# Token rows in a region of DRAM per expert, scattered in three rounds, and the gates computed inside the first expert

## The reference: what is computed

```python
new_re = ar * S_re - ai * S_im
new_im = ar * S_im + ai * S_re
kv = np.einsum('bhd,bhe->bhde', k[:, :, t], v[:, :, t])
S_re, S_im = (new_re + kv, new_im)
y[:, :, t] = np.einsum('bhd,bhde->bhe', q[:, :, t], S_re)
```

```python
expert_idx = np.argmax(logits, axis=1)
...
for i in range(N):
    e = expert_idx[i]
    if counts[e] < capacity:
        disp[e, counts[e]] = x[i]
        pos[i] = counts[e]
        counts[e] += 1
        keep[i] = True
h = np.maximum(np.einsum('ecd,edf->ecf', disp, w1), 0.0)
y = np.einsum('ecf,efd->ecd', h, w2)
```

## Time and profile before

| | |
|---|---|
| median of 3 runs | 549.45 us (549.38 to 549.66) |
| the profiled execution | 548.02 us, span 546.1 us |
| TensorE, products | 467.5 us busy, 86% of the span |
| TensorE, weight loads | 417.7 us, 76% |
| VectorE | 363.7 us, 67% |
| ScalarE | 272.3 us, 50% |
| GpSimd | 42.9 us, 8% |
| moved by DMA | 63.69 MB, mean 117 GB/s |
| mean granted clock of TensorE | 0.952 |

### The profile page before, as it was taken

The page is one execution under the profiler, slowest core; times in us unless marked ns, Lnnn a source line. Parts: engine busy times, 40 slices in busy tenths (PEclk is TensorE's granted clock), DMA queues, the critical chain, the costliest instruction groups (busy, mean ns, idle before and its releaser), DMA issues.

```text
span 546.1 us, 10002 instructions
## 1 busy us (share of the span) xinstructions
PE 467.5 (86%) x3752; PEld 417.7 (76%) x3752; DVE 363.7 (67%) x624; ACT 272.3 (50%) x431; POOL 42.9 (8%) x48
## 2 busy tenths in 40 slices
PE   0538976999996029999999999999999999999995
PEld 0237755777885029999999998989998899889985
DVE  2688798678534317776777776778747787487751
ACT  5996758673446017666666664433334333334212
POOL 2000000000001890000000000000002000110002
PEclk9959999999998559999999999999999999999999
DMA  8970000000000469667666666233324333230001
GB/s 323 424 294 2 3 1 1 2 1 2 2 3 2 159 188 324 182 192 215 205 195 199 200 189 190 89 99 104 96 78 145 102 101 114 70 108 0 1 0 60
DMA packets 22178, 63.69 MB, mean 117 GB/s; under 512 B 2928, under 2 KB 4464, under 8 KB 22128
## 3 DMA queue, kind: packets, MB, share of 16 engines
q1 hardware_dynamic: 20592, 58.27, 32.6%
q0 software_dynamic: 1536, 4.74, 2.3%
HBM read 58.27 MB, written 4.74 MB: 115 GB/s over the span
## 4 chain that ended last, share of the span: by engine, by line
PE 74%; DVE 8%; DMA 5%; issue 5%; POOL 3%; ACT 2%; SPq 2%; DVEq 0%; POOLq 0%; ACTq 0%
PE banks L1152 15%; PE banks L1150 15%; PE banks L1151 15%; PE banks L1160 7%; DMA vv<-v_rows 4%; PE banks L1161 3%; PE banks L998 3%; POOL rows_by_slot L369 3%; PE banks L986 2%; PE banks L1017 2%; PE banks L989 2%; PE banks L950 2%; PE banks L1020 1%; PE banks L1144 1%; PE banks L1046 1%
## 5 line engine op out<-in xcount | busy, mean ns | idle before, releaser
L870 DVE TENSOR_TENSOR w_lo<-raw_early,w_hi 128x768 fp32r<-128x768 f32 x84 | 80.0, 956 | 31.1 <-ACT w_hi L543 30.0
L588 ACT ACTIVATE g_hi<-g_all 128x512 fp32r<-128x512 f32 x48 | 30.3, 632 | 118.4 <-DVE g_all L923 118.4
L543 ACT ACTIVATE w_hi<-raw_early 128x768 fp32r<-128x768 f32 x84 | 70.4, 843 | 33.2 <-PE banks L1161 32.7
L1150 PE MATMUL banks<-w_hi,g_hi 128*128 128x384 f32 x192 | 65.1, 339 | 0.5 <-DVE g_lo L925 0.5
L1152 PE MATMUL banks<-w_hi,g_lo 128*128 128x384 f32 x192 | 65.0, 339 | 0.0
L1151 PE MATMUL banks<-w_lo,g_hi 128*128 128x384 f32 x192 | 64.9, 338 | 0.0
L1160 PE MATMUL banks<-h_hi_lo,w_hi 128*128 128x448 f32 x192 | 64.0, 378 | 0.9 <-DVE h_hi_lo L886 0.9
L925 DVE TENSOR_TENSOR g_lo<-g_all,g_hi 128x512 fp32r<-128x512 f32 x48 | 33.3, 693 | 44.2 <-ACT g_hi L588 44.2
L1150 PE MATMUL banks<-ys_hi,w_hi 128*128 128x512 f32 x144 | 56.1, 390 | 1.2 <-DVE ys_lo L900 1.2
L1152 PE MATMUL banks<-ys_hi,w_lo 128*128 128x512 f32 x144 | 57.1, 397 | 0.0
L1151 PE MATMUL banks<-ys_lo,w_hi 128*128 128x512 f32 x144 | 56.8, 394 | 0.0
(11 more groups left out here) (166 smaller groups left out, 981.2 us busy)
## 6 DMA issues: line engine op xcount, KB each, us to landing
raw_early<-weights SPq DMA_DIRECT2D x84, 384.0 KB, 3.5
raw_late<-weights SPq DMA_DIRECT2D x28, 384.0 KB, 3.5
xq<-q_rows SPq DMA_DIRECT2D x3, 776.0 KB, 16.6
xq<-rows_by_slot SPq DMA_DIRECT2D x12, 194.0 KB, 4.5
kk<-k_rows SPq DMA_DIRECT2D x3, 768.0 KB, 18.0
vv<-v_rows SPq DMA_DIRECT2D x3, 768.0 KB, 19.4
aa<-a_re_rows SPq DMA_DIRECT2D x2, 768.0 KB, 10.5
th<-a_im_rows SPq DMA_DIRECT2D x2, 768.0 KB, 11.9
```

Of the source, the lines that this page charges most:

```text
L543: A(wh[:, slot, :], raw[slot], ACT.Copy).then_inc(w_hi, 1)
L588: A(gh[:, c % GBUF, :], gg[:, c % GBUF, :], ACT.Copy).then_inc(g_hi, 1)
L870: TT(wl[:, slot, :], raw[slot], wh[:, slot, :].bitcast(F32), ALU.subtract).then_inc(w_lo, 1)
L1150: MM(o, lhsT=whi, rhs=mhi, start=first, stop=False)
```

## The change

**Regions.** In DRAM each expert has a region of 1536 rows (`rows_by_expert`), its middle at row 768 of the region. Tokens of batch 0 are placed downwards from the middle and those of batch 1 upwards, so a token's place follows from its rank within its own batch, block by block, and later blocks don't move it. A window of 384 rows (`CAP`) that begins at the region's first used row, but at most 384 ahead of the middle, holds an expert's tokens.

**Zeros.** Rows in reach of a window must be defined: SyncE, after the loads of attention, copies the still all-zero `w0` to 768 rows in each region (8 transfers of 1.18 MB); `shift_state` waits for them, and so does the first scatter.

**Rounds.** `ROUNDS` cuts the six blocks into (0 to 3), (4), (5), that is tiles 0 to 7, 8 and 9, 10 and 11. `choose(r)` and `place(r)` on VectorE and `rank(r)` on TensorE do a round; the first two are put at steps 5 to 8 of the last frame, the third behind it. `X_IN` and `LOGITS_IN` place transposes and logits anew. GpSimd scatters each round's tiles when `routed` says so.

**Windows.** SyncE loads the first window in three parts, then chunks 6 and 7 of the weights, then windows 1 and 2; a further window ahead of each expert's weights. Two tiles of a window (256 rows) are turned and split: those of expert 0 ahead of the experts, those of e+1 inside expert e (TensorE after outputs 1 and 4, ScalarE and VectorE at chunks 3 and 6). The third tile is used by wide experts only.

**Gates.** Only `choose`, `place`, the region's ends, starts and flags stand between the last logits and the experts. The slot in sorted order, keep and gate weight are made by `gate_part(i)` in chunks 0 to 5 of expert 0 on VectorE. Gate and token number leave the rows (now 384 wide) and go through a DRAM array of two values a slot (`meta_by_slot`), scattered by twelve small transfers and loaded back at expert 4.

**Also.** Three of the six first weight splits come ahead of the first window, three behind; the memsets of `ys_hi` and `ys_lo` follow the last scatter; the results of the experts use four banks in turn instead of five.

```diff
+    FIRST = 3
+    WB = 4
+    MID = S
+    REGION = S + S
+    WT = CAP // P
+    NTILES = 2
+    ZT = 8
+    PADE = E // 2
+    ROUNDS = ((0, NB - 2), (NB - 2, NB - 1), (NB - 1, NB))
...
+        X_IN = {2: ((0,), (1,), (2,)), 3: ((3,), (4,), (5,)), 4: ((6,), (7,), ()), 5: ((), (), (8,)),
+                7: ((9,), (), ()), 8: ((), (), (10,)), 10: ((11,), (), ())}
+        LOGITS_IN = {2: ((), (0,), (1,)), 3: ((2,), (3,), (4,)), 4: ((5,), (6,), (7,)),
+                     6: ((), (), (8,)), 7: ((), (9,), ()), 9: ((10,), (), ())}
         assert NT == 12
+        NEXT_FROM = (1, 4)
+        NEXT_AT = (3, 6)
...
-            sp.wait_ge(bases, 1)
+            sp.wait_ge(consts, 1)
+            for e in range(E):
+                sp.dma_start(xs_dram[e * REGION + MID - CAP:e * REGION + MID + CAP, :].rearrange(
+                    "(p t) w -> p t w", t=ZT), w0[0:2 * CAP // ZT, None, 0:UW].to_broadcast([2 * CAP // ZT, ZT, UW])
+                    ).then_inc(zeroed, 16)
+
+            def window_row(e):
+                return sp.value_load(start_i[0:1, e:e + 1], min_val=0, max_val=E * REGION - CAP)
+
+            def window_rows(row, lo, n):
+                return xs_dram[bass.ds(row, CAP), :].rearrange("(t p) w -> p t w", p=P)[:, lo:lo + n, :]
+
+            def load_window(e, row):
+                sp.dma_start(win[:, e % WB, :, :], window_rows(row, 0, WT)).then_inc(win_dma[e], 16)
+
+            sp.wait_ge(windows, 1)
+            start_rows = [window_row(e) for e in range(FIRST)]
+            sp.wait_ge(scattered, 16 * NT)
+            for t in range(WT):
+                sp.dma_start(win[:, 0, t, :], window_rows(start_rows[0], t, 1)[:, 0, :]).then_inc(first_dma[t], 16)
             for i in range(AHEAD, RING):
                 sp.dma_start(raw[i], w_in[i, :, :]).then_inc(w_dma[i], 16)
-
-            sp.wait_ge(scattered, 16 * NT)
-            for r in range(0, NT, LOAD_ROWS):
-                sp.dma_start(orow[:, r:r + LOAD_ROWS, :],
-                             xs_dram[r * P:(r + LOAD_ROWS) * P, :].rearrange("(t p) w -> p t w", p=P)
-                             ).then_inc(row_dma[r // LOAD_ROWS], 16)
+            for e in range(1, FIRST):
+                load_window(e, start_rows[e])
...
-            with sp.Fori(1, E) as e:
+            for e in range(1, E):
+                if FIRST - 1 < e + FIRST - 1 < E:
+
+                    sp.wait_ge(used, USED_FREE + RING * max(e + FIRST - WB, 0))
+                    load_window(e + FIRST - 1, window_row(e + FIRST - 1))
                 for i in range(RING):
                     load_chunk(RING * e + i, RING * e + (i + 1 - RING), i)
+                if e == E // 2:
+                    sp.wait_ge(meta_scattered, 16 * NT)
+                    sp.dma_start(meta[:, :, :], meta_dram.rearrange("(t p) w -> p t w", p=P)).then_inc(meta_dma, 16)
...
+            pool.wait_ge(zeroed, 16 * E)
+            for r, (n0, n1) in enumerate(ROUNDS):
+                pool.wait_ge(routed, r + 1)
+                for t in range(B * n0, B * n1):
+                    pool.indirect_dma_start(xs_dram, bass.IndirectOffsetOnAxis(ap=slots_i[:, t:t + 1], axis=0),
+                                            xq[:, t * UW:(t + 1) * UW], None).then_inc(scattered, 16)
+            pool.wait_ge(bases, 1)
             pool.memset(yh[:, :, :].bitcast(F32), 0.0)
             pool.memset(yl[:, :, :].bitcast(F32), 0.0).then_inc(cleared, 1)
+
+            pool.wait_ge(meta_ready, 1)
+            for t in range(NT):
+                pool.indirect_dma_start(meta_dram, bass.IndirectOffsetOnAxis(ap=comp_i[:, t:t + 1], axis=0),
+                                        meta_src[:, t, :], None).then_inc(meta_scattered, 16)
...
+            act.wait_ge(logits_made, XT_FREE + NT)
+            for i in range(FIRST):
+                split_hi(i, i, 1)
...
+                    dve.wait_ge(zeroed, 16 * E)
...
+            def choose(r):
+
+                n0, n1 = ROUNDS[r]
+                T = slice(B * n0, B * n1)
+                n = B * (n1 - n0)
+                dve.wait_ge(logits_made, XT_FREE + B * n1)
+                source = LB[:, T.start * E:T.stop * E].rearrange("p (t e) -> p t e", e=E)
+                if r + 1 < len(ROUNDS):
+                    dve.tensor_copy(logit[:, T, :], source).then_inc(logits_out, 1)
+                    dve.wait_ge(logits_out, r + 1)
+                    source = logit[:, T, :]
+                then(dve.tensor_reduce(top[:, T], source, AX_X, ALU.max))
+                then(TT(rt[:, 0, T, :], source, wide(top[:, T], n), ALU.is_equal))
+                then(TT(rt[:, 0, T, :], rt[:, 0, T, :], prior[:, None, :].to_broadcast([P, n, E]), ALU.mult))
+                then(dve.tensor_reduce(best[:, T], rt[:, 0, T, :], AX_X, ALU.max))
+                if n > B:
+                    then(TT(rt[:, 0, T, :], rt[:, 0, T, :], wide(best[:, T], n), ALU.is_equal))
+                    TT(one_hot[:, T, :].rearrange("p (n b) e -> p n b e", b=B),
+                       rt[:, 0, T, :].rearrange("p (n b) e -> p n b e", b=B),
+                       sign[:, None, :, :].to_broadcast([P, n1 - n0, B, E]), ALU.mult).then_inc(onehot, 1)
+                else:
+                    STT(one_hot[:, T.start, :], rt[:, 0, T.start, :], best[:, T.start:T.start + 1], sign[:, 0, :],
+                        ALU.is_equal, ALU.mult)
+                    STT(one_hot[:, T.start + 1, :], rt[:, 0, T.start + 1, :], best[:, T.start + 1:T.stop], sign[:, 1, :],
+                        ALU.is_equal, ALU.mult).then_inc(onehot, 1)
+                dve.wait_ge(onehot, r + 1)
+                for m in range(n0, n1):
+                    TT(before[:, m + 1, :, :], before[:, m, :, :], one_hot[:, B * m:B * m + B, :], ALU.add
+                       ).then_inc(prefixed, 1)
+                    if m + 1 < n1:
+                        dve.wait_ge(prefixed, m + 1)
+
+            def place(r):
+
+                n0, n1 = ROUNDS[r]
+                T = slice(B * n0, B * n1)
+                dve.wait_ge(ranked, r + 1)
+                TT(rt[:, 0, T, :], RK[r][:, 0:B * (n1 - n0) * E].rearrange("p (t e) -> p t e", e=E),
+                   one_hot[:, T, :], ALU.mult).then_inc(ranks_read, 1)
+                dve.wait_ge(ranks_read, r + 1)
+                then(dve.tensor_reduce(slot[:, T], rt[:, 0, T, :], AX_X, ALU.add))
+                TT(slots_i[:, T].rearrange("p (n b) -> p n b", b=B), slot[:, T].rearrange("p (n b) -> p n b", b=B),
+                   sign[:, None, :, 0].to_broadcast([P, n1 - n0, B]), ALU.mult).then_inc(routed, 1)
...
+            choose(2)
+            place(2)
+
+            dve.wait_ge(summed, 1)
+            then(dve.tensor_copy(ends[:, :, :], ENDS[:, 0:B * E].rearrange("p (b e) -> p b e", b=B)))
+            TT(start_i[0:1, :], ends[0:1, 0, :], low[0:1, :], ALU.max).then_inc(windows, 1)
+            then(STT(count, ends[:, 1, :], 1.0, ends[:, 0, :], ALU.add, ALU.subtract))
+            TS(wide_i[0:1, :], count[0:1, :], float(NARROW), float(WIDE), ALU.is_gt, ALU.mult).then_inc(flags, 1)
+            TS(wide_f[0:1, :], count[0:1, :], float(NARROW), float(WIDE), ALU.is_gt, ALU.mult)
+            for i in range(3):
+                then(TT(steps_of[:, i + 1, PADE:PADE + E], steps_of[:, i, PADE:PADE + E],
+                        steps_of[:, i, PADE - (1 << i):PADE + E - (1 << i)], ALU.add))
...
+            for i in range(FIRST):
+                split_lo(i, i)
...
+                if i == 0:
+                    step(1, TT(move[:, :], first, start[:, :], ALU.subtract))
+                    step(2, of_token(move[:, :]))
+                    step(3, dve.tensor_reduce(mine, rt[:, 0, :, :], AX_X, ALU.add))
...
+                if i == 5:
+                    step(15, STT(total, total, 1e-9, ones[:, 0:NT], ALU.add, ALU.mult))
+                    step(16, dve.reciprocal(gate, total))
+                    dve.tensor_copy(meta_src[:, :, 1], tok_id[:, :])
+                    TT(meta_src[:, :, 0], gate, keep, ALU.mult).then_inc(meta_ready, 1)
...
+            for t in range(NTILES):
+                window_lo(0, t)
...
+                        if e == 0:
+                            gate_part(i)
+                        if i in NEXT_AT and e + 1 < E:
+                            window_lo(e + 1, NEXT_AT.index(i))
...
+            def rank(r):
+
+                n0, n1 = ROUNDS[r]
+                to = RK[r][:, 0:B * (n1 - n0) * E]
+                if r == 1:
+                    pe.wait_ge(state_out, U_FREE + 6 * (NF - 1) + 2)
+                pe.wait_ge(ranks_read, r)
+                pe.wait_ge(prefixed, n1 - 1)
+                MM(to, lhsT=ones[:, :], rhs=before[:, n0:n1, :, :].rearrange("p n b e -> p (n b e)"), start=True, stop=False)
+                pe.wait_ge(onehot, r + 1)
+                MM(to, lhsT=upto[:, :], rhs=one_hot[:, B * n0:B * n1, :].rearrange("p t e -> p (t e)"),
+                   start=False, stop=True).then_inc(ranked, 1)
...
+            def tile_T(e, t):
+                if e == 0:
```

(100 more changed lines are left out.)

273 lines of the change are left out of this document (136 added, 137 removed).

## The result

The changed kernel takes 554.26 us (median of 20 runs, 549.25 to 557.77) against 549.33 (20 runs, 547.53 to 550.12): ratio 1.0075, 95% interval 1.0053 to 1.0097. It is slower by 4.9 us where I had forecast 16.7 faster. The profiled run took 554.28 us, span 552.5.

The account below looks back on a forecast made before the run. TensorE was taken to bound attention, experts and MLP, with one large hole between attention and first expert. Gain 24.2, less 1.9 clock, 4.2 window turning, 1.4 output delay: 16.7 off 549.45 gives 532.8 us, range 530 to 535 (all cases 529 to 543).

Parts of the forecast that it names:

- The hole: Between last logits and first expert product: two scatters left instead of twelve, product at 184.6 instead of 208.82, 24.2 us gained.
- Nothing waits for either: Twelve scatters of eight bytes a row from about 195 and the result tiles' memsets hold nothing up: no cost.
- tail of attention: End of attention: two pairs of extra rank products and moved logits delay the last logits by 1.3 us, between 0 and 3.
- The other side's mechanism: The slower case: zeros landing late hold up the first turn of the state at 80.70; at 149 GB/s +20.1 us.
- rival 1: After the logits: the last scatter falls behind VectorE's splits again, +3.2 us, 536.0; 20%.
- In the experts: Window tiles turned inside TensorE's stream cost 4.2 us, pushed output 1.4 us; experts 16.8 us apart from the second on.
- Expert 0 with gates and slow clock: First expert: TensorE needs 18.1 us, including 1.9 lost to half clock; VectorE's gates and splits add 0, at most 2.
- DMA, zeros: ScalarE may wait 1 us for chunk 8, covered by lead; zeros written by 70, before 80.70: no cost.
- rival 3: Zeros late before the state's first turn at 80.70: at 149 GB/s +20.1 us, 552.9; 5%.
- Rivals 2 and 4: Windows dearer in the experts, +7, 540, 12%; round one waits late in attention, most scatters after the logits, 543, 4%.
- The sum: Whole kernel: 24.2 - 1.9 - 4.2 - 1.4 = 16.7 us gained, from 549.45 to 532.8 us.
- The chances: Whole kernel: faster 0.94, same 0.01, slower 0.05; own case 59%.

Follow-up runs that it names:

- the first of group 5: The changed kernel with each small scatter in the experts waiting for the landing of the one before, and their rows' load moved into the MLP: 536.74 us.
- the third of group 4: The changed kernel with each small scatter, left in the experts, waiting for the landing of the one before: 541.72 us.

## Why the prediction was wrong, step by step

- **What bounds it**: right. The hole and TensorE set the time after, too.
- **The failed step** is the cost of scatters *beside* TensorE. I moved ten of them under attention and counted there only the rank products and VectorE's two early rounds, and I wrote of the small ones and memsets "Nothing waits for either". Nothing does wait for them; with them TensorE's signals and its issue are held up all the same: +10.9 us and +7.3 us. My +1.3 (0 to 3) for the tail of attention was 14.4 in the changed kernel (186.00 - 171.56). The earlier trace rows had no scatter with TensorE at work, so their cost beside attention or an expert had no row; I bounded dearer waits, but not this. The other side's mechanism was looked for in the zeros. The trace of before has scatters beside TensorE only in the MLP, four in a row from here on, and TensorE was busy through all of 409 to 415:

```profile
409.19 0.97 POOL L377 DMA_INDIRECT out_rows<-xq,tok_slot  x1 [203.05 <-ACT xq L597]
```

- **Tail of attention**, +1.3 (0 to 3): in the six traces where attention didn't stall the last logits come at 173.87 to 175.13 and not 172.9, so +2.3 to +3.6 on 171.56: dearer than forecast, and at the edge of the bounds.
- **The hole**: right. 11.8 us from last logits to first expert product, forecast 11.7; no blocked scatter, rival 1 didn't happen.
- **In the experts**: 16.84 us each ((324.68 - 206.80) / 7 in the first of group 5), forecast 16.8. Expert 0 with gates and slow clock: 20.0 us to its results (186.84 to 206.80), against 15.4 before and my 18.1, so 1.9 dearer. Of that 0.8 are TensorE's waits for VectorE's half of h, which I had at 0 (at most 2), and some 0.4 the clock; the rest isn't resolved. The clock was at half until about 191.4, 4.6 us behind the first product, so 2.3 us by my way of counting, forecast 1.9.
- **DMA, zeros**: no wait at 81.50, rival 3 false. ScalarE waited 2.88 us for chunk 8 (until 195.57 in the first of group 5), where I had 1; TensorE's next wait was 0.2. Rivals 2 and 4 didn't happen either.
- **The sum**: where no row stalls, the change gives 536.5 to 536.7, a gain of 12.3 to 12.5 us. Of the 16.7, 2.2 went in the tail and 1.9 in expert 0. With 536.6 + 10.9 + 7.3 one is at 554.8; measured 554.26.
- **The chances**: 5% for slower was too sure. All of it stood on one named mechanism, while the change set 22 instructions of a kind beside short, dense products, where the trace had never shown them. That the time came out near the kernel before is no sign of a small error: 12.3 to 12.5 gained and some 18 lost.

## What to carry to other kernels

An indexed DMA of GpSimd isn't free just because nothing waits for it. Before moving a row of them beside dense TensorE work, look for a stretch of the trace that shows the two together; if there is none, price the move on the chip with a few dummy ones. Keep them apart in time, or put them where a trial shows no loss (here the MLP; whether its long products are the reason no run tells), and judge such a kernel by several executions on several chips. Where VectorE operations with two inputs from SBUF meet a run of scatters on the critical path, it can pay to hold them back: until the last scatter was issued, it was worth 4.2 us here.

## What was unexpected in the hardware

- Eight scatters of 8-byte rows cost 6.1 us (555.07 - 548.97), as much as eight of 1536 bytes (5.5 us); eight plain DMAs of 1536-byte rows by the same engine cost nothing.
- During a stall what comes from TensorE is late: 1.9 to 5.1 us from a product's end to its signal in attention, and 6.2 us in expert 1, where products that end at 225.92 are taken up by ScalarE at 232.12. No signal of ScalarE or VectorE to TensorE was seen to come late: TensorE's 3.74 us ahead of 169.20 are put down to ScalarE's own late start. The ends of products are modelled in a trace, so a product that really ended late would look the same.
- Two kernels whose engines did the same at the same instants, within 0.02 us over the 30 us ahead of the first scatter, parted behind it: the last logits came 23.96 us after that scatter in the changed kernel and 12.51 us in the third of group 4.
